# Second expert's rows gathered by quarters and turned by VectorE in a fused attention, gated layer and top-2 expert kernel

## The chip, the cores and the metric

One core of one Trainium2 chip runs the whole program in one launch. The metric is device time in microseconds (us), the median of several executions. The engines are TensorE (PE, with its weight loads as PEld), VectorE (DVE), ScalarE (ACT), GpSimd (POOL) and SyncE (SP), which here only issues transfers. Each runs its own instruction list in order; they meet at semaphores.

## What is computed

```python
x = attention(q, k, v)                      # window 64, 2304 rows of 512
x = (sigmoid(x @ w_gate) * (x @ w_val)) @ w_out
logits = x @ moe2_w_gate + log1p(exp(x @ moe2_w_noise)) * noise
top2 = the two largest of 8 logits, weights by softmax of the two
for e in range(8):                          # w1[e]: 512x1024, w2[e]: 1024x512
    out[rows of e] += weight * (relu(x[rows of e] @ w1[e]) @ w2[e])
```

## The kernel before, in words

Every float32 product is made of three TensorE products. Each operand is split into a high part, rounded by ScalarE, and a low part, the rest, subtracted by VectorE, and high by high, high by low and low by high are added up in PSUM.

The first stage (some 520 us) does the attention and the gated layer in 9 groups of 256 rows and 12 chunks each (GROUPS, FC; LAST is 108 chunks). The router decides for each group which rows go to which expert; GpSimd writes each row's number and weight into the table `places` in DRAM (`place_rows`).

The second stage goes over 8 experts (e). An expert has room for 5 tiles of 128 rows (TILES): tiles 0 to 2 are half p = 0 (368 columns are used), tiles 3 and 4 half p = 1 (256). What doesn't fit goes into left-over tiles after all experts. For each expert TensorE runs `up(e, p, f)` for 8 chunks f of 128 hidden columns (12 matmuls each), and `down(e, a)` for 5 tiles a (24 matmuls each). After each `up`, ScalarE's `relu` (line 1384) makes the high part of the hidden chunk, VectorE's `hidden_low` (L1732) the low part; `up(f)` needs the `hidden_low` of chunk f - 2, since two PSUM banks alternate. After each `down`, ScalarE's `rows_out` (L1394) scales the tile by the row weights, and GpSimd's `scatter` (L793) adds it to `out`.

An expert's weights come in 8 units of 128x1024 (n = 0 to 3 is w1, 4 to 7 is w2) through 4 raw buffers. SyncE loads them (`load_expert`), ScalarE's `high` (L1362) and VectorE's `low` (L1711) split them. There are two copies of the split w1 and one of w2: units 4 to 7 of expert 1 may be written only after the last `down` of expert 0, and the first `down` of expert 1 waits for all 8 (`e_lo`).

The rows of a tile are gathered by GpSimd with an indirect transfer (`gather(n)`) into one of two buffers `x_g`, and have to be turned, columns to partitions. There are two ways:

- Tiles of experts 0 and 1 (n < SQUARES = 10): one gather of whole rows (L779), then `turn_g(n)` on TensorE, four 128x128 transposes into PSUM (L1086). `xt_high` (L1374) and `xt_low` (L1725) split them from there.
- Tiles of experts 2 to 7: four gathers of quarter rows (L774), one for each quarter of the tile's rows, by a table `tab_q` whose row numbers VectorE has turned into quarter numbers (L1836 to L1838). VectorE's `turn_rows(n)` (L1719) transposes 32x32 blocks into the SBUF tile `x_t` (`v_nat1`). The w1 of such an expert is loaded by four transfers a unit (L577), so that its rows stand in the matching order.

The first two experts are interleaved. The order of the tiles is `ORDER = [0, 1, 2, 5, 6, 7, 3, 4, 8, 9]`, then 10 and on, where tile number is 5e + a; n counts places in this order. TensorE's list from the end of the first stage is `up(0,0)`, then `turn_g(3)`, `down(0,0)`, `turn_g(4)`, `down(0,1)`, `turn_g(5)`, `down(0,2)`; `up(1,0)` with `turn_g(6)` after f = 4 and `turn_g(7)` after f = 6; `up(0,1)`; `turn_g(8)`, `down(0,3)`, `turn_g(9)`, `down(0,4)`; `up(1,1)`; five `down(1,a)`; and from expert 2 on `up(e,0)`, `up(e,1)` and five `down` in turn. The orders on the other engines are written out by hand in the same way. During `up(1,1)` units 4 to 7 of expert 1 are split after f = 0, 2, 4 and 6. Before it VectorE works out the count of left-over tiles, a chain of 17 small instructions (L1846 to L1864).

GpSimd's list around this place: `place_rows(7)`, `gather(3)`, `gather(4)`; after the loop `place_rows(8)` (the last group), `gather(5)`, `scatter(0)`, `gather(6)`, `scatter(1)`, `gather(7)`, `scatter(2)`, `gather(8)`, `gather(9)`, `gather(10)`, `scatter(3)`, and so on. `gather(n)` waits until tile n - 2 is turned; `gather(5)` waits for the store of the last group's rows, which SyncE issues (`store_y`, L563) once gathers 0 to 4 have landed.

Of the kernel before, what the change touches and what calls it, by code (L numbers as in the profile page):

```python
# [13 lines left out]
P = 128  # L14


def attention_two_moe_program(nc, q, k, v, gv, w_out, r_gate, r_noise, noise, w1, w2, out):
# [61 lines left out]
    SQUARES = AHEAD * TILES  # L79
# [8 lines left out]
    UNITS = 8  # L88
    UW = 2 * EXW // UNITS
# [6 lines left out]
    with ExitStack() as ctx:  # L96
# [36 lines left out]
        tab_q = shared[:, 0:8 * (NE - AHEAD) * TILES].bitcast(I32).rearrange("p (b e n w) -> p b e n w", b=4, n=TILES, w=2)  # L133
# [38 lines left out]
        quarter = sb("quarter", [P, 1], I32)  # L172
        idx_r = sb("idx_r", [P, 1], I32)
# [168 lines left out]
        tab_q_in = sem("tab_q_in")  # L342
        quarters_done = sem("quarters_done")
# [30 lines left out]
        def turned_at(n):  # L374

            return ps_xt.rearrange("p (k m) -> p k m", k=KC) if n < SQUARES else x_t

        def turn_no(m):
            return ORDER.index(m)

        def loads(q):

            return 16 * sum(4 if i // UNITS >= AHEAD and i % UNITS < KC else 1 for i in range(q % 4, q + 1, 4))

        def gathers(n):

            return 16 * sum(1 if i < SQUARES else 4 for i in range(n % 2, n + 1, 2))

# [119 lines left out]
        def _(sp):  # L508
# [99 lines left out]
            for s in range(LAST + 2):  # L608
# [46 lines left out]
            for u in range(2):  # L655
                sp.wait_ge(gathered[u], 16 * ((5 + 1 - u) // 2))
# [3 lines left out]
            by_quarter = places.rearrange("(b c e n) w -> c b e (n w)", b=4, c=Q4, e=NE)[:, :, AHEAD:NE, 0:2 * TILES]  # L660
# [15 lines left out]
        def _(pool):  # L676
# [78 lines left out]
            def gather(n):  # L755
# [12 lines left out]
                if n >= SQUARES:  # L768
                    if n == SQUARES:
                        pool.wait_ge(quarters_done, 1)  # L770
                    pool.nop(nofuse=True)
                    e, a = divmod(m, TILES)
                    for b in range(4):
                        pool.indirect_dma_start(x_g[:, n % 2, b * P:(b + 1) * P], None, x2_quarters,  # L774
                                                bass.IndirectOffsetOnAxis(tab_q[:, b, e - AHEAD, a, 0:1], 0)
                                                ).then_inc(gathered[n % 2], 16)
# [57 lines left out]

            place_rows(GROUPS - 1)
            gather(5)
# [42 lines left out]
        def _(pe):  # L879
# [318 lines left out]
            for a in range(HEAD):  # L1198
                turn_g(3 + a)
# [7 lines left out]
            turn_g(8)  # L1207
            down(0, 3)
            turn_g(9)
# [38 lines left out]
        def _(act):  # L1248
# [679 lines left out]
```

## Time and profile before

| | |
|---|---|
| median of 3 runs | 983.2 us (982.27 to 983.57) |
| the profiled execution | 981.25 us |
| its span, first to last instruction | 979.0 us |
| TensorE busy | 968.5 us, 99% of the span |
| VectorE, ScalarE, GpSimd busy | 512.5, 370.1, 400.1 us |
| granted TensorE clock, mean | 0.999 of full |

The profile is of one execution. Its own time, 981.25 us, is the span and 2.25 us around it; the runs that are compared by their median are other executions. The chain of waits is followed back from the last instruction: a piece of it that is not a matmul is time in which TensorE stood still for somebody. A timeline row is one instruction, or several of a kind in a row, with the idle time of the engine before it in brackets, and what ended it. Ends of matmuls are modelled: consecutive pieces overlap by some 0.16 us in the timeline, not in the chain.

### The profile page before, as it was taken

Reading aid. Unit: us, or ns where it says so; the run is one execution under the profiler, and the core shown is the slowest. Engines: PE = TensorE matmul, PEld = TensorE weight load, DVE = VectorE, ACT = ScalarE, POOL = GpSimd, SP = SyncE. Lnnn points to the kernel's source line nnn. Section 1 sums busy time; section 2 is a strip of 40 time slices with the busy share of each in tenths; the row PEclk is TensorE's granted clock in tenths of the full one; section 3 lists DMA queues with packets and bytes.
Section 4 is the critical chain, followed back from the end, with each engine's and each line's share of the span. In section 5 each row is a group of like instructions: output and inputs, shape, how many; then the busy total and the mean of one; then the engine's idle time right before and its main releaser. Section 6 shows DMA issues by size and latency. Waiting matters only on the chain.

```text
span 979.0 us, 17644 instructions
## 1 busy us (share of the span) xinstructions
PE 968.5 (99%) x6503; PEld 853.5 (87%) x6503; DVE 512.5 (52%) x1277; ACT 370.1 (38%) x892; POOL 400.1 (41%) x401
## 2 busy tenths in 40 slices
PE   8999999999999999999999999999999999999997
PEld 7998888888888888888999898798998989898995
DVE  5565576665757576664554535543534434443420
ACT  6553343433334343423244423343433334343411
POOL 4882224242332424331212414663828284664402
PEclk9999999999999999999999999999999999999999
DMA  6756333243534324232044443672636466482503
GB/s 223 230 177 167 118 112 107 89 141 94 149 99 133 103 72 135 77 97 86 23 119 130 56 128 75 167 166 74 154 85 139 109 150 129 114 165 76 96 2 52
DMA packets 82727, 113.09 MB, mean 116 GB/s; under 512 B 19216, under 2 KB 45840, under 8 KB 82640
## 3 DMA queue, kind: packets, MB, share of 16 engines
q1 hardware_dynamic: 69008, 84.63, 29.5%
q0 software_dynamic: 13344, 27.05, 13.9%
q8 instruction: 53, 0.87, 0.4%
q14 instruction: 34, 0.28, 0.1%
q10 hardware_dynamic: 288, 0.26, 0.1%
HBM read 83.13 MB, written 28.77 MB: 114 GB/s over the span
## 4 chain that ended last, share of the span: by engine, by line
PE 98%; issue 0%; ACT 0%; DVE 0%; POOL 0%; POOLq 0%; ACTq 0%
PE bank L1118 22%; PE bank L1102 22%; PE bank L995 16%; PE bank L1018 16%; PE bank L1001 10%; PE bank L999 5%; PE bank L975 2%; PE bank L913 2%; PE bank L1125 1%; PE bank L1086 0%; PE bank L1044 0%; PE bank L1053 0%; PE bank L931 0%; PE bank L1066 0%; DVE wr L1711 0%
## 5 line engine op out<-in xcount | busy, mean ns | idle before, releaser
L1001 PE MATMUL bank<-xr,wr 128*128 128x256 f32 x864 | 242.7, 281 | 0.0
L995 PE MATMUL bank<-xr,wr 128*128 128x512 f32 x672 | 240.2, 397 | 0.0
L1102 PE MATMUL bank<-wr 128*128 128x256 f32 (+1 forms) x1536 | 223.6, 306 | 0.6 <-DVE xr L1732 0.5
L1102 PEld LDWEIGHTS bank<-wr 128*128 128x128 f32 x1536 | 221.1, 190 | 2.1 <-DVE xr L1732 1.0
L774 POOL DMA_INDIRECT arena<-x_rows,shared x120 | 129.7, 1081 | 145.6 <-DVE v_nat L1719 97.4
L1018 PE MATMUL bank<-wr,hr 128*128 128x512 f32 x648 | 170.6, 398 | 0.0
L742 POOL TENSOR_TENSOR hr<-arena,hr 128x256 fp32r<-128x256 f32 x84 | 62.0, 738 | 263.7 <-ACT hr L1315 263.7
L1001 PEld LDWEIGHTS bank<-xr,wr 128*128 128x128 f32 x864 | 163.6, 189 | 3.4
L995 PEld LDWEIGHTS bank<-xr,wr 128*128 128x128 f32 x672 | 126.2, 188 | 30.3
L1018 PEld LDWEIGHTS bank<-wr,hr 128*128 128x128 f32 x648 | 114.0, 188 | 23.3 <-issue 0.2
L1118 PE MATMUL bank<-wr 128*128 128x512 f32 (+1 forms) x576 | 133.2, 391 | 0.9 <-DVE wr L1711 0.9
L1118 PEld LDWEIGHTS bank<-wr 128*128 128x128 f32 (+1 forms) x576 | 104.9, 183 | 25.8 <-DVE wr L1711 1.1
L1315 ACT CAST hr<-arena 128x256 fp32r<-128x256 f32 x108 | 43.9, 407 | 133.3 <-DVE arena L1603 129.5
L1588 DVE TENSOR_REDUCE arena<-bank 128x256 f32<-128x512 f32 x84 | 58.1, 692 | 63.2 <-PE bank L1001 57.8
L1118 PE MATMUL bank<-wr,xr 128*128 128x512 f32 x384 | 88.8, 390 | 0.0
L1711 DVE TENSOR_TENSOR wr<-arena,wr 128x1024 fp32r<-128x1024 f32 x64 | 77.2, 1210 | 15.4 <-ACT wr L1362 11.3
L1118 PEld LDWEIGHTS bank<-wr,xr 128*128 128x128 f32 x384 | 71.9, 188 | 15.0
L1593 DVE TENSOR_REDUCE arena<-bank 128x256 f32<-128x512 f32 x84 | 58.0, 691 | 47.8 <-PE bank L1001 44.8
L1308 ACT ACTIVATE arena<-arena 128x256 f32<-128x256 f32 x84 | 35.0, 416 | 125.8 <-DVE arena L1588 125.3
L793 POOL DMA_INDIRECT out<-arena,tab x34 | 56.4, 1659 | 58.2 <-ACT arena L1394 51.2
L1394 ACT ACTIVATE arena<-bank,tab 128x512 f32<-128x512 f32 (+1 forms) x34 | 23.5, 690 | 133.7 <-PE bank L1118 106.8
L999 PE MATMUL bank<-xr,wr 128*128 128x256 f32 x384 | 70.1, 283 | 0.4 <-issue 0.4
(158 smaller groups left out, 1022.2 us busy)
## 6 DMA issues: line engine op xcount, KB each, us to landing
arena<-moe_w SPq DMA_DIRECT2D x40, 512.0 KB
arena<-moe_w SPq DMA_DIRECT2D x96, 128.0 KB
p_rows<-arena SPq DMA_DIRECT2D x28, 256.0 KB, 2.0
v_nat<-p_rows SPq DMA_DIRECT2D x112, 64.0 KB
arena<-gv SPq DMA_DIRECT2D x12, 512.0 KB, 4.5
out<-zeros POOLq DMA_DIRECT2D x20, 256.0 KB, 2.8
x_rows<-arena SPq DMA_DIRECT2D x9, 512.0 KB, 3.8
arena<-k SPq DMA_DIRECT2D x17, 256.0 KB, 4.9
```

What stands on the lines that cost most here:

```text
L742: pool.tensor_tensor(hr[:, r, 1], gate[:, 0], hr[:, r, 0].bitcast(F32), ALU.subtract).then_inc(h_lo, 1)
L774: pool.indirect_dma_start(x_g[:, n % 2, b * P:(b + 1) * P], None, x2_quarters, bass.IndirectOffsetOnAxis(tab_q[:, b, e - AHEAD, a, 0:1], 0 ...
L793: pool.indirect_dma_start(out[:, :], bass.IndirectOffsetOnAxis(row_no(m)[0:n], 0), y_s[0:n, m % 2], None, compute_op=ALU.add).then_inc(sca ...
L995: pe.matmul(ps_g[m].rearrange("p (a n) -> p a n", a=2), gv_w[:, f, m, kk], xr[:, g % 2, :, kk], start=(kk == 0), stop=False, skip_group_ch ...
L999: pe.matmul(ps_g[m][:, 0:GT], gv_w[:, f, m, kk], xr[:, g % 2, x, kk], start=(kk + x == 0), stop=False, skip_group_check=True)
L1001: mm = pe.matmul(ps_g[m][:, 0:GT], gv_w[:, f, 2 + m, kk], xr[:, g % 2, 0, kk], start=False, stop=(kk == KC - 1), skip_group_check=True)
L1018: mm = pe.matmul(ps_y[t], hr[:, f % 2, a, t * P:(t + 1) * P], wo_w[:, b, f], start=(f == 0 and n == 0), stop=(f == FC - 1 and n == 2))
L1102: mm = pe.matmul(ps_h[u % 2][:, 0:n], w1_r[e % 2][:, a, kk, f * P:(f + 1) * P], xT[p][:, b, kk, 0:n], start=(kk + x == 0), stop=(kk == KC ...
L1118: mm = pe.matmul(ps_e[m % 2][0:n], hT[p][:, i, f, cols.start:cols.start + n], w2_r[:, j, f], start=(f + x == 0), stop=(f == F2C - 1 and x ...
L1588: dve.tensor_reduce(gate[:, 0], ps_g[0].rearrange("p (a n) -> p n a", a=2), AX.X, ALU.add).then_inc(gates_added, 1)
L1593: dve.tensor_reduce(gate[:, 1], ps_g[1].rearrange("p (a n) -> p n a", a=2), AX.X, ALU.add).then_inc(vals_added, 1)
L1711: dve.tensor_tensor(unit(e, n, 1), raw[:, n % 4], unit(e, n, 0).bitcast(F32), ALU.subtract).then_inc(e_lo, 1)
```

## The change

Expert 1's tiles too now go the way of experts 2 to 7: quarter gathers, `turn_rows` on VectorE, w1 loaded by quarters. `SQUARES` becomes the first expert of this kind, and `squared(n)` tells which places in the order are meant: n = 3, 4, 5, 8, 9. The row numbers of its first three tiles come early in a table of their own, by four more transfers, and VectorE turns them into quarter numbers in chunk LAST - 5. `gather(5)` moves ahead of `place_rows(8)`. The rest of the quarter numbers is made one loop of 8 `hidden_low` earlier, and `gather(8)` waits for it. The left-over count moves behind the whole of VectorE's expert work. The last units of expert 1's weights are split after f = 0, 1, 3 and 5, and in every expert from 1 on ScalarE runs `xt_high` of the next expert's tile ahead of `rows_out`. For e = 0 and tiles 3 and 4 (n = 6, 7) nothing changes.

```diff
-    SQUARES = AHEAD * TILES
+    SQUARES = 1
+    LAST_UNITS = [0, 1, 3, 5]
+        tab_q_first = sb("tab_q_first", [P, 4, HEAD, 2], I32)
         def turned_at(n):
-            return ps_xt.rearrange("p (k m) -> p k m", k=KC) if n < SQUARES else x_t
+            return x_t if squared(n) else ps_xt.rearrange("p (k m) -> p k m", k=KC)
+        def squared(n):
+            return ORDER[n] // TILES >= SQUARES
@@ load_expert @@
-                if n < KC and e >= AHEAD:
+                if n < KC and e >= SQUARES:
@@ SyncE @@
+                    for j in range(4):
+                        sp.dma_start(tab_q_first[j * Q4:(j + 1) * Q4].rearrange("p b n w -> p b (n w)"),
+                                     places.rearrange("(b c e n) w -> c b e (n w)", b=4, c=Q4, e=NE)[:, :, SQUARES, 0:2 * HEAD]
+                                     ).then_inc(tab_q_first_in, 16)
                     for n in range(4, UNITS):
                         load_expert(0, n)
...
             for u in range(2):
-                sp.wait_ge(gathered[u], 16 * ((5 + 1 - u) // 2))
+                sp.wait_ge(gathered[u], gathers(4 - u))
             store_y(GROUPS - 1)
...
-            by_quarter = places.rearrange("(b c e n) w -> c b e (n w)", b=4, c=Q4, e=NE)[:, :, AHEAD:NE, 0:2 * TILES]
+            by_quarter = places.rearrange("(b c e n) w -> c b e (n w)", b=4, c=Q4, e=NE)[:, :, SQUARES:NE, 0:2 * TILES]
@@ GpSimd, gather(n) @@
-                if n >= SQUARES:
-                    if n == SQUARES:
+                if squared(n):
+                    if n == HEAD:
+                        pool.wait_ge(quarters_first, 1)
+                    if n == AHEAD * HEAD + LATE:
                         pool.wait_ge(quarters_done, 1)
                     pool.nop(nofuse=True)
                     e, a = divmod(m, TILES)
                     for b in range(4):
+                        no = tab_q_first[:, b, a, 0:1] if is_early(m) else tab_q[:, b, e - SQUARES, a, 0:1]
...
+            gather(5)
             place_rows(GROUPS - 1)
-            gather(5)
             scatter(0)
@@ TensorE @@
             for a in range(HEAD):
-                turn_g(3 + a)
                 down(0, a)
...
             for f in range(F2C):
                 up(0, 1, f)
-            turn_g(8)
             down(0, 3)
-            turn_g(9)
             down(0, 4)
@@ ScalarE @@
-                if f % 2 == 0:
-                    high(1, KC + f // 2)
+                if f in LAST_UNITS:
+                    high(1, KC + LAST_UNITS.index(f))
             for a in range(TILES):
                 if a < KC:
                     high(AHEAD, a)
+                xt_high(AHEAD * TILES + a)
                 rows_out(1, a)
-                xt_high(SQUARES + a)
...
                     if e < NE - 1 and a < KC:
                         high(e + 1, a)
-                    rows_out(e, a)
                     if e < NE - 1:
                         xt_high(TILES * (e + 1) + a)
+                    rows_out(e, a)
@@ VectorE @@
             def turn_rows(n):
                 dve.wait_ge(gathered[n % 2], gathers(n))
-                if n > SQUARES:
-                    dve.wait_ge(xt_hi, n)
-                    dve.wait_ge(xt_lo, n)
+                dve.wait_ge(xt_hi, n)
+                dve.wait_ge(xt_lo, n)
...
+                if s == LAST - 5:
+                    dve.wait_ge(tab_q_first_in, 16 * 4)
+                    link(dve.tensor_scalar(quarter[:], quarter[:], 5, None, ALU.arith_shift_right))
+                    to_quarters(tab_q_first[:].rearrange("p b n w -> p (b n) w")[:, :, 0]).then_inc(quarters_first, 1)
...
             hidden_low(0, 0, 2)
+            turn_rows(HEAD)
             copy_logits(GROUPS - 1)
...
             for a in range(HEAD):
-                xt_low(3 + a)
+                xt_low(HEAD + a)
+                if a + 1 < HEAD:
+                    turn_rows(HEAD + a + 1)
                 low(1, a)
...
                 hidden_low(1, 0, f)
                 if f in (4, 6):
                     xt_low(f // 2 + 4)
+            dve.wait_ge(tab_q_in, 16 * 16)
+            to_quarters(tab_q[:].rearrange("p b e n w -> p (b e n) w")[:, :, 0]).then_inc(quarters_done, 1)
             for f in range(F2C):
                 hidden_low(0, 1, f)
+                if f == 4:
+                    turn_rows(8)
-            dve.wait_ge(tab_q_in, 16 * 16)
-            link(dve.tensor_scalar(quarter[:], quarter[:], 5, None, ALU.arith_shift_right))
...
             xt_low(8)
+            turn_rows(9)
             xt_low(9)
...
             for f in range(F2C):
                 hidden_low(1, 1, f)
-                if f % 2 == 0:
-                    low(1, KC + f // 2)
+                if f in LAST_UNITS:
+                    low(1, KC + LAST_UNITS.index(f))
```

## Rows read from the trace of the kernel before

**Rows 1.** The page: the chain that ended last, by engine
```profile
PE 98%; issue 0%; ACT 0%; DVE 0%; POOL 0%; POOLq 0%; ACTq 0%
```

**Rows 2.** The chain in order of time: start us, us, what
```profile
544.40 0.44 PE bank L1086 x4
...
562.17 10.00 PE bank L1102 x60
...
596.91 5.51 PE bank L1118 x24
...
643.43 27.51 PE bank L1102 x192
...
945.11 27.29 PE bank L1118 x120
```

**Rows 3.** Timeline of TensorE: start us, us, instruction, idle before
```profile
576.82 13.75 PE L1102 MATMUL bank<-wr 128*128 128x368 f32 x108
...
602.25 4.47 PE L1102 MATMUL bank<-wr 128*128 128x256 f32 x36
...
615.89 16.67 PE L1118 MATMUL bank<-wr 128*128 128x512 f32 x72 [0.88 <-DVE wr L1711]
```

**Rows 4.** Timeline of ScalarE in up(1,1)
```profile
603.88 0.38 ACT L1384 ACTIVATE xr<-bank 128x256 fp32r<-128x256 f32 x1 [0.74 <-issue]
604.16 1.04 ACT L1362 CAST wr<-arena 128x1024 fp32r<-128x1024 f32 x1
606.28 0.38 ACT L1384 ACTIVATE xr<-bank 128x256 fp32r<-128x256 f32 x1 [1.08 <-PE bank L1102]
```

**Rows 5.** Timeline of VectorE in up(1,1)
```profile
604.29 0.42 DVE L1732 SCALAR_TENSOR_TENSOR xr<-bank,xr 128x256 fp32r<-128x256 f32 x1 [0.51 <-ACT xr L1384]
605.23 1.23 DVE L1711 TENSOR_TENSOR wr<-arena,wr 128x1024 fp32r<-128x1024 f32 x1 [0.51 <-issue]
...
614.61 1.22 DVE L1711 TENSOR_TENSOR wr<-arena,wr 128x1024 fp32r<-128x1024 f32 x1 [0.51 <-ACT wr L1362]
```

**Rows 6.** Timeline of VectorE from expert 0's first downs to the left-over count
```profile
559.56 1.22 DVE L1711 TENSOR_TENSOR wr<-arena,wr 128x1024 fp32r<-128x1024 f32 x1
...
579.61 0.54 DVE L1732 SCALAR_TENSOR_TENSOR wr<-bank,wr 128x368 fp32r<-128x368 f32 x1 [1.19 <-ACT wr L1384]
...
586.70 0.42 DVE L1732 SCALAR_TENSOR_TENSOR xr<-bank,xr 128x256 fp32r<-128x256 f32 x1 [1.01 <-ACT xr L1384]
...
591.54 0.29 DVE L1838 SCALAR_TENSOR_TENSOR shared<-shared,quarter 128x120 int32<-128x120 int32 x1
...
598.32 0.16 DVE L1846 CAST arena<-steps_i 128x14 f32<-128x14 int32 x1
```

**Rows 7.** Timeline of GpSimd: gathers and the last group's places
```profile
518.42 0.99 POOL L779 DMA_INDIRECT arena<-x_rows,tab_first  x1 [0.30 <-issue]
...
546.61 1.01 POOL L752 DMA_INDIRECT places<-pairs,slot_i  x1 [25.31 <-DVE pairs L1697]
...
592.57 0.95 POOL L774 DMA_INDIRECT arena<-x_rows,shared  x1 [13.77 <-DVE shared L1838]
...
596.32 0.95 POOL L774 DMA_INDIRECT arena<-x_rows,shared  x1 [0.30 <-issue]
...
637.67 0.95 POOL L774 DMA_INDIRECT arena<-x_rows,shared  x1 [0.30 <-issue]
...
651.30 1.67 POOL L774 DMA_INDIRECT arena<-x_rows,shared  x1 [0.30 <-issue]
```

**Rows 8.** Timeline of VectorE: the turn of expert 2's last tile
```profile
641.19 0.71 DVE L1719 STREAM_TRANSPOSE v_nat<-arena 128x512 f32<-128x512 f32 x1 [1.24 <-DMA arena<-x_rows,shared]
```

**Rows 9.** Busy time by stretch: us, PE, PEld, DVE, ACT, POOL, clock, DMA share, GB/s
```profile
598.60:600.00 1.40, 1.40 (x8) 1.15 (x7) 1.23 (x6) 0.00 (x0) 1.10 (x2) 1.00 0.00 0
```

**Rows 10.** Timeline of SyncE, and the page's landing time of such a store
```profile
529.36 0.38 SPq L563 DMA_DIRECT2D x_rows<-arena  x1
...
x_rows<-arena SPq DMA_DIRECT2D x9, 512.0 KB, 3.8
```

More of the change, by code:

```diff
@@ L342, in attention_two_moe_program @@
         tab_q_in = sem("tab_q_in")
+        tab_q_first_in = sem("tab_q_first_in")
+        quarters_first = sem("quarters_first")
         quarters_done = sem("quarters_done")
@@ L1711, in low, with to_quarters @@
                 dve.tensor_tensor(unit(e, n, 1), raw[:, n % 4], unit(e, n, 0).bitcast(F32), ALU.subtract).then_inc(e_lo, 1)
+            def to_quarters(numbers):
+                return dve.scalar_tensor_tensor(out=numbers, in0=numbers, scalar=4.0,
+                                                in1=quarter[:].broadcast_to(list(numbers.shape)), op0=ALU.mult, op1=ALU.add)
             def turn_rows(n):
                 dve.wait_ge(gathered[n % 2], gathers(n))
-                if n > SQUARES:
-                    dve.wait_ge(xt_hi, n)
-                    dve.wait_ge(xt_lo, n)
+                dve.wait_ge(xt_hi, n)
+                dve.wait_ge(xt_lo, n)
                 dve.nop(nofuse=True)
@@ L1830, in _ @@
                     xt_low(f // 2 + 4)
+            dve.wait_ge(tab_q_in, 16 * 16)
+            to_quarters(tab_q[:].rearrange("p b e n w -> p (b e n) w")[:, :, 0]).then_inc(quarters_done, 1)
             for f in range(F2C):
                 hidden_low(0, 1, f)
-            dve.wait_ge(tab_q_in, 16 * 16)
-            link(dve.tensor_scalar(quarter[:], quarter[:], 5, None, ALU.arith_shift_right))
-            q_rows = tab_q[:].rearrange("p b e n w -> p (b e n) w")[:, :, 0]
-            dve.scalar_tensor_tensor(out=q_rows, in0=q_rows, scalar=4.0, in1=quarter[:].broadcast_to([P, 4 * (NE - AHEAD) * TILES]),
-                                     op0=ALU.mult, op1=ALU.add).then_inc(quarters_done, 1)
+                if f == 4:
+                    turn_rows(8)
             xt_low(8)
+            turn_rows(9)
             xt_low(9)
+            for f in range(F2C):
+                hidden_low(1, 1, f)
+                if f in LAST_UNITS:
+                    low(1, KC + LAST_UNITS.index(f))
+            for a in range(TILES):
+                turn_rows(AHEAD * TILES + a)
+                if a < KC:
+                    low(AHEAD, a)
+                xt_low(AHEAD * TILES + a)
+            for e in range(AHEAD, NE):
+                for p in range(2):
+                    for f in range(F2C):
+                        hidden_low(e, p, f)
+                        if p == 0 and f < KC:
+                            low(e, KC + f)
+                for a in range(TILES):
+                    if e < NE - 1:
+                        turn_rows(TILES * (e + 1) + a)
+                    if e < NE - 1 and a < KC:
+                        low(e + 1, a)
+                    if e < NE - 1:
+                        xt_low(TILES * (e + 1) + a)
             rem, before, upto, share = (left[:, i] for i in range(4))
```

29 lines of the change are left out of this document (4 added, 25 removed).

## The prediction

> **What bounds the kernel.** I read the page's chain first: 98% of it is TensorE [rows 1]. A stall removed elsewhere is worth nothing; only TensorE's own work and its stops count. Then the chain in order of time around the change. From expert 2 on there is nothing to win: a half plus half of `up` takes 27.51 us and five `down` 27.29 us [rows 2], the same every time, so a matmul of 512 columns goes at 0.227 us, one `down` of 24 at 5.46, an `up` chunk of p = 1 at 1.44 (three in 4.47, with the 0.16 by which a timeline piece overlaps the next [rows 3]) and of p = 0 at (27.51 - 8 x 1.44) / 8 = 2.0. Third, TensorE's timeline of the one place that is slower than this: `up(1,1)` begins at 602.25 and the `down` behind it at 615.89 [rows 3], 13.64 us for eight chunks that need 11.52. So 2.12 us are lost there, 0.88 of them waiting for the last `low`. The clock is granted in full (0.999), and the engine is busy before and after the change alike, so I leave it there.
>
> **The change, part by part.**
>
> *Five turns leave TensorE.* From 544.40 to 562.17 stand three turns and three `down` [rows 2]: 17.77 - 3 x 5.46 = 1.39 us. From 590.57, the end of the piece that begins at 576.82 [rows 3], to 602.42, the end of the second `down` [rows 2], stand two and two: 11.85 - 10.92 = 0.93. Together 2.3 us (by the row of one turn, 0.44, it would be 2.2). All of it is on the path. `up(1,0)`, `up(0,1)` come 1.4 us earlier, `up(1,1)` 2.3.
>
> *The last units of expert 1 at f = 0, 1, 3, 5.* I run the same row durations forward, counting from the first matmul of `up(1,1)`. `relu(f)` starts 0.19 behind the end of its chunk, at 1.63 for f = 0; `high` 0.28 later and takes 1.04 [rows 4]; `hidden_low` starts 0.41 after `relu` and takes 0.44, `low` 1.23 [rows 5]. `low` of unit 4 then ends at 4.21, `hidden_low(1)` behind it at 4.57, so chunk 3, due at 4.32, starts at 4.61. Unit 5 ends at 5.7 and costs nothing. Unit 6 ends at 8.8, `hidden_low(4)` at 9.18, so chunk 6, due at 8.95 by then, starts at 9.22. Unit 7 ends at 11.72, before the last chunk does at 12.10. The first `down` starts at 12.1 in place of 13.64: 1.5 us. Both ends: 2.1 if no stop is left, and 0.9 if `relu(1)` is late again as it is now (606.28, where 605.3 was due by the chunks [rows 4]; what held it the trace does not say), since that shifts the same run to 12.77. I take 1.5, by the durations of the rows.
>
> *Gathers 3, 4 and 5 in four parts.* Four issues take 3 x 1.25 + 0.95 = 4.7 us (592.57 and 596.32 are the first and fourth), 0.3 apart from the next; in the dearest row one takes 1.67 [rows 7]. Gather 3 starts at 518.42 as before; gathers 3 and 4 are out by 528.4, or by 534 at 1.97 a part. SyncE issues sixteen loads for w1 where there were four, and four small table loads; then the store that stood at 529.36 and lands in 3.8 us [rows 10] goes at 531 to 537. `gather(5)` behind it is out by 540 to 549. Behind `gather(5)` GpSimd now has `place_rows(8)`, due at 546.61 [rows 7]: at worst 2 us late. What waits for that is the table, then `gather(6)`, needed by `turn_g(6)` at 572.17 - 1.4 [rows 2], 24 us after: four writes of 1.3, a table transfer and a gather at 3.8 each at most leave some 10 us. Nothing.
>
> *VectorE's turns*, 0.71 each [rows 8]. `turn_rows(4)` and `(5)` stand in waits for ScalarE's `rows_out`. What they must not delay is `low(1,3)`: it ended at 560.78 [rows 6] with `up(1,0)` at 562.17; it hangs on `down(0,1)`, which ends 0.93 us earlier, so 559.85 against 560.8 with 0.9 us left. `turn_rows(3)` and `(9)` have several us each. Nothing.
>
> *`gather(8)` and `turn_rows(8)`* is the tight place, since VectorE waits for the transfer with `hidden_low(0,1,5)` behind it, and TensorE's last chunk behind that. `hidden_low(1,0,7)` starts at 579.61 - 1.4 = 578.2 [rows 6], the quarter numbers are done at 579.05, GpSimd follows 0.74 later as it does now (591.83 to 592.57 [rows 6, 7]), the fourth issue ends at 584.5. Landing: at most 1.3 us later by one row (issue ended at 597.27, no traffic from 598.60 [rows 7, 9]), 2.6 by another, with other transfers beside it (issue ended at 638.62, turn released at 641.19 [rows 7, 8]). So 585.8 to 587.1. `turn_rows(8)` is due at 586.70 + 0.42 - 1.4 + 0.2 = 585.9 [rows 6]; TensorE's chunk 7 starts at 590.57 - 1.44 - 1.4 = 587.7, so a landing by 586.5 costs nothing and one at 587.1 costs 0.6. I take nothing: at 580 to 590 no weights are loading (the next load waits for `low(1,4)`), as in the row with 1.3.
>
> *The left-over count*, some 6 us (598.32 to 604.29 [rows 5, 6]), ended just in time for the first `hidden_low` of `up(1,1)`. It now runs from about 945, when TensorE begins its last 27.29 us [rows 2]; GpSimd asks for it ahead of the last but one scatter, some 20 us on. Nothing either way. *ScalarE's `xt_high` ahead of `rows_out`*: the fifth turn ends at 641.90 [rows 8], the copy by 642.6 if it takes as long, `down(1,4)` at 643.43 [rows 2]. Nothing, and nothing to gain, since these stages have no stop.
>
> Sum: 2.3 + 1.5 = 3.8 to 3.9 us. The profiled execution took 981.25 us (span 979.0 and 2.25 around it) and would take 977.4; the median of the runs, 983.2, lies 1.95 above it, so I say 979.3. A difference under 0.2%, 2 us, could not be told from none.
>
> **Rivals.**
>
> *The stop in `up(1,1)` stays* (0.15). Two units follow each other at f = 0 and 1, where VectorE has 1.23 + 0.44 = 1.67 us of work a chunk against TensorE's 1.44. With `relu(1)` late again it is 979.9; if all 2.1 us stay, 983.2 - 2.3 = 980.9.
>
> *`gather(8)` lands late* (0.08). For it: an issue of 1.67 with 0.3 behind it exists [rows 7]. Four such end at 587.4, landing at 590.0, 3.5 us past 586.5: 982.8. Against it: that row lies beside a `low`, and there is none at 580 to 585. The Trainium skill (GPSIMD Engine Reference, Specifications) says that GpSimd shares its SBUF interface with VectorE instructions that have two SBUF inputs, which a `low` has and a `hidden_low` has not; by that rule the long issues would stay away here, and the trace agrees so far, with 1.67 us beside a `low` and 0.95 without one.
>
> *VectorE's turns come onto the path* (0.03). If TensorE waited for each, 5 x 0.71 = 3.6 us would take the place of 2.3: 983.2 + 1.2 - 1.5 = 982.9. Against it: each has at least 0.9 us to spare above. The Trainium skill (VectorE: DVE Perf Modes, Rules for kernel authors) advises TensorE for a 128x128 transpose where PSUM will do as its target; by that advice the change would be given up and the 2.3 us stay in, and the time would be 981.7. The row speaks both ways: 0.71 us is longer than 0.44, but on an engine that is half idle.
>
> *Slower: `rows_out` held by `xt_high` in every expert* (0.05). ScalarE now waits for the fifth gather of the next expert before it frees a PSUM bank and starts the next `relu`. From the landing, turn, copy and `rows_out` (0.71 each at most), `relu` 0.4 and `hidden_low` 0.54 must end by chunk 2 of the next `up`, 643.43 + 4.0; from 641.19 [rows 2, 8] that leaves 3.1 us. If the gather lands 4.6 us later than now, 1.5 us are lost in each of six experts: 983.2 - 3.9 + 9 = 988.3. It decides from 4.1 us on (six times 1.0). Against it: GpSimd's order there is unchanged and its work moves with TensorE.
>
> *The change does not do what it says* (0.03): if the turns stayed on TensorE, 983.2 less what the units bring, 981.7. The five calls are gone from its list.
>
> **Numbers.** The forecast has 0.66. Its own range is 978.7 (no stop left) to 980.2. The stop's rival reaches 980.9, half of the late gather 981.1; runs of one kernel spread by 0.7 us. 978.2 to 981.6 leaves out the full late gather, the VectorE rival and the slower one. Faster by over 0.2% (under 981.2): the forecast, the first rival nearly whole and part of the second, 0.81. Within: the rest of these, the third and the last, 0.14. Slower: 0.05.
>
> **What would show it.** No L1086 between 544 and 562 but `down` after `down` at 5.46, `up(1,0)` at 560.8; two `down` of 10.9 before `up(1,1)` at 599.9; 12.1 us from there to the next `down`, at 612.0, with pauses of 0.3 before chunks 3 and 6; `turn_rows(8)` at 586, at once followed by `hidden_low`; the stages from expert 2 on at 27.51 and 27.29. Wrong would be a stop of TensorE at 587.7, or `down(1,0)` after 613, or a stage of a later expert over 27.6.

## The result: slower in the recorded measurement, faster on half of the chips

| | before | after | ratio, 95% interval |
|---|---|---|---|
| recorded measurement, median us | 982.93 (982.24 to 983.57, 6 runs) | 991.12 (989.66 to 992.82, 6 runs) | 1.0091 [1.0078, 1.0103] |
| its profiled execution: us, span, clock | 981.25, 979.0, 0.999 | 992.82, 991.1, 0.992 | |
| chip 2 | 980.97 | 977.53 | 0.9968 [0.9956, 0.998] |
| chip 2, a second time | 980.79 | 976.81 | 0.9962 [0.9949, 0.9976] |
| chip 8 | 980.59 | 976.83 | 0.9959 [0.9939, 0.9978] |
| chip 3 | 986.07 | 997.12 | 1.0098 [1.0072, 1.0124] |

The prediction, 979.3 us, missed the recorded time by 12 us. The same kernel, unchanged, then ran on other chips, and there it stands either 3.4 to 4.0 us below the kernel before, as forecast, or 11 above it. So two questions have to be kept apart: what the edits bring, and what some chips take. (The numbers only tell the chips apart; that of the recorded measurement is not on record.)

**Where the time went in the recorded profile.** The chain in order of time of the changed kernel (start us, us, what):

```profile
525.85 5.91 issue
531.77 4.02 PE bank L1118 x12
535.79 2.25 PE bank L1034 x6
538.04 2.00 PE bank L1118 x12
...
554.93 16.39 PE bank L1134 x72
571.32 10.00 PE bank L1118 x60
...
598.52 3.28 issue
601.79 2.45 PE bank L1118 x12
604.25 11.68 PE bank L1134 x48
...
628.20 27.34 PE bank L1134 x120
```

What was forecast is there: three `down` without a turn between them take 16.39 (17.77 with the turns, [rows 2]), and the stages from 628.20 on are as before. But TensorE stops twice, for 5.91 us ahead of the first chunk of `up(0,0)` and for 3.28 ahead of the last chunk of `up(0,1)`, and behind each stop the same work is slow. Busy time by stretch, the columns as in [rows 9] (us, PE, PEld, DVE, ACT, POOL, clock, DMA share, GB/s):

```profile
526.00:531.70 5.70, 0.00 (x0) 0.00 (x0) 0.00 (x0) 0.38 (x1) 3.07 (x4) 0.91 0.84 209
531.70:538.00 6.30, 6.23 (x19) 5.79 (x20) 3.21 (x4) 2.30 (x3) 0.00 (x0) 0.54 0.28 87
598.60:601.70 3.10, 0.00 (x0) 0.00 (x0) 0.38 (x1) 0.38 (x1) 2.19 (x4) 1.00 0.14 42
601.70:606.00 4.30, 4.21 (x17) 3.80 (x18) 0.04 (x1) 0.00 (x0) 2.72 (x3) 0.60 0.20 60
```

The granted clock falls to the 1.2 GHz level once TensorE has stood still: 12 matmuls of 368 columns in 4.02 us where 2.00 is usual, the last chunk of `up(0,1)` in 2.45 where 1.44 is, and the two `down` in 11.68 where 10.91 is. The first stop costs 5.91 + 2.02 + 0.86 = 8.8 us, the second 3.28 + 1.01 + 0.77 = 5.1. Together 13.9 us; less the 3.8 forecast that is 10.1, where the medians differ by 8.2 and the two profiled executions by 11.6 (the profiled one of after also waits 1.8 us for a load at its start).

**What the stops wait for.** In both, ScalarE, VectorE and TensorE nearly stand still and move on together; of the engines only GpSimd works all the time, and issues gathers. In the first stop the sixteen loads of w1 run as well (DMA share 0.84), in the second hardly anything does (0.14), so those loads can't be what both have in common. GpSimd's timeline, the last of the 12 issues in a row of the first place (four `place_rows`, gathers 3 and 4), then of the 12 of the second place the first of gather 8 and the fourth of gathers 8, 9 and 10:

```profile
529.03 0.95 POOL L791 DMA_INDIRECT arena<-x_rows,tab_q_first  x1 [0.30 <-issue]
...
590.26 1.00 POOL L791 DMA_INDIRECT arena<-x_rows,shared  x1 [15.87 <-DVE shared L1729]
...
594.08 0.94 POOL L791 DMA_INDIRECT arena<-x_rows,shared  x1 [0.30 <-issue]
...
599.09 0.95 POOL L791 DMA_INDIRECT arena<-x_rows,shared  x1 [0.30 <-issue]
...
604.09 0.95 POOL L791 DMA_INDIRECT arena<-x_rows,shared  x1 [0.30 <-issue]
```

And ScalarE's timeline, the gate of the first place and the `relu` of the second:

```profile
531.24 0.38 ACT L1321 ACTIVATE arena<-bank 128x256 f32<-128x256 f32 x1 [7.42 <-issue]
...
595.92 0.39 ACT L1397 ACTIVATE xr<-bank 128x256 fp32r<-128x256 f32 x1 [1.55 <-PE bank L1118]
600.90 0.38 ACT L1397 ACTIVATE xr<-bank 128x256 fp32r<-128x256 f32 x1 [4.59 <-remote]
607.26 0.66 ACT L1397 ACTIVATE xr<-bank 128x256 fp32r<-128x256 f32 x2 [5.97 <-remote]
```

The `relu` at 607.26 handles two chunks at once. TensorE had ended the first of them at 598.52 (the chain above), 8.7 us earlier; the second ended at 604.25. The one at 600.90 belongs to the chunk before, done at 596.8. So TensorE's work was finished, and its semaphore increments reached the other engines late.

The trace settles that it is the increment and not ScalarE that is late, since it holds each change of a semaphore with its own time. The chunks that ended at 596.82, 598.52 and 604.25 changed theirs at 600.88, 607.24 and 607.36. Counted over whole programs, the traces of the recorded measurement (before and after) and of chips 1, 3 and 11 each hold 9 to 27 changes made by TensorE, of some 640, that come 0.1 us or more behind the end of the matmul; the traces of chips 2, 6 and 8 hold none, of 663. No change made by ScalarE or VectorE is that late in any trace, on either kind of chip. And each late one falls into a run of GpSimd's issues or within 3 us of its end. The kernel before has them too in the recorded measurement, up to 1.9 us late around its `place_rows` and gather 3.

At the second place the increments arrive about when a gather is through: the fourth issues of the three gathers end at 595.0, 600.0 and 605.0, the `relu` follow at 595.9, 600.9 and 607.3. At the first place it is the same with the gate of the last chunk of the feed-forward layer: TensorE is done with it by 524.5, ScalarE starts at 531.24, and the run of issues ends at 529.98; the first chunk of `up(0,0)` starts 0.5 us after the gate. At the second place `up(f)` needs `hidden_low(f - 2)`, which needs the increment. A chunk takes 1.44 us, and `relu` and `hidden_low` are through some 0.9 behind its end, so TensorE stands still as soon as an increment is more than some 0.5 us late.

This calls a row of the kernel before in question. `relu(1)` at 606.28 [rows 4], for a chunk that ended at 605.3, is a late increment too, just behind the four issues of a gather.

### The profile page after: what moved, and what is told of

Its sections match the earlier page's. It is cut to its first block, busy times and chain, and to the rows that moved or that the text cites. A ratio compares the mean times of both kernels' runs of the same rounds, so it can differ in the third digit from the quotient of the medians.

```text
span 991.1 us, 17647 instructions
## 1 busy us (share of the span) xinstructions
PE 971.0 (98%) x6483; PEld 855.4 (86%) x6483; DVE 516.0 (52%) x1283; ACT 372.1 (38%) x892; POOL 423.7 (43%) x416
## 4 chain that ended last, share of the span: by engine, by line
PE 97%; issue 1%; DMA 1%; ACT 0%; POOL 0%; SPq 0%; DVE 0%; POOLq 0%
PE bank L1118 23%; PE bank L1134 22%; PE bank L1011 16%; PE bank L1034 16%; PE bank L1017 10%; PE bank L1015 5%; PE bank L991 2%; PE bank L929 2%; DMA arena<-q 1%; PE bank L947 0%; PE bank L1060 0%; PE bank L1069 0%; PE bank L1082 0%; PE bank L1141 0%; PE bank L1102 0%
## 5 line engine op out<-in xcount | busy, mean ns | idle before, releaser
L1118 PE MATMUL bank<-wr 128*128 128x256 f32 (+1 forms) x1536 | 226.5, 308 | 9.4 <-issue 9.2
L1118 PEld LDWEIGHTS bank<-wr 128*128 128x128 f32 x1536 | 223.5, 191 | 11.4 <-issue 10.3
L791 POOL DMA_INDIRECT arena<-x_rows,shared x128 | 139.7, 1091 | 140.3 <-DVE v_nat L1737 87.6
L809 POOL DMA_INDIRECT out<-arena,tab x34 | 62.5, 1837 | 64.0 <-ACT arena L1407 55.8
L1750 DVE SCALAR_TENSOR_TENSOR wr<-bank,wr 128x368 fp32r<-128x368 f32 x64 | 34.5, 539 | 64.7 <-ACT wr L1397 54.2
```

Source lines behind the costliest of these rows:

```text
L809: pool.indirect_dma_start(out[:, :], bass.IndirectOffsetOnAxis(row_no(m)[0:n], 0), y_s[0:n, m % 2], None, compute_op=ALU.add).then_inc(sca ...
L1118: mm = pe.matmul(ps_h[u % 2][:, 0:n], w1_r[e % 2][:, a, kk, f * P:(f + 1) * P], xT[p][:, b, kk, 0:n], start=(kk + x == 0), stop=(kk == KC ...
```

## The experiments

Times are given as the kernel's median against the median of the kernel before on the same chip, in us, with the ratio and its interval.

### Three versions without the long runs of issues (chip 6)

`e1_whole_all` takes gathers 3, 4, 5, 8 and 9 of the changed kernel as one transfer each, `e2_whole_first` 3, 4 and 5; `e4_paced`, called the paced kernel below, keeps all parts and holds them apart.

```diff
                     pool.nop(nofuse=True)
+                    if n in (3, 4, 5, 8, 9):
+                        pool.indirect_dma_start(x_g[:, n % 2], None, x2_rows[:, :], bass.IndirectOffsetOnAxis(row_no(m), 0)
+                                                ).then_inc(gathered[n % 2], 16)
+                        return
                     e, a = divmod(m, TILES)
```

```diff
                 if s == LAST - 2:
+                    pool.wait_ge(up_done, 2)
                     gather(4)
...
-            for n in (8, 9, 10):
-                gather(n)
+            gather(8)
+            pool.wait_ge(up_done, F2C * (half_no(0, 1) + 1))
+            gather(9)
             scatter(3)
+            gather(10)
```

> The changed kernel, with gathers 3, 4, 5, 8 and 9 as one transfer each in place of four (VectorE still turns them, w1 of expert 1 is still loaded by quarters). Left out: the rows of expert 1 then stand in another order than its w1, so its part of the output is not the reference's; the work of every other engine is the same. Theory A (a long run of GpSimd's indirect transfers, 12 without a pause, holds back the increments of TensorE's semaphores, and TensorE stops): both stops go, and the turns and the better order stay won: about 979. Rival B (the stops come from the sixteen w1 loads, or from the order of ScalarE and VectorE): the time stays near 991. Rival C (a dip of the granted clock that is there anyway, and the stop follows it): near 991.

> The same for gathers 3, 4 and 5 alone; 8 and 9 stay in four parts (the rows of three tiles of expert 1 then stand in another order than its w1: their part of the output is not the reference's). Theory A: the first stop (525.85 to 531.77 and the slow clock behind it, some 8 us) goes, the second (598.52 to 601.79, and the slow clock behind it, some 5 us) stays: 983 to 985. Rivals B and C: 991.

> The changed kernel with all its transfers, but broken up: gather 4 waits until TensorE has done two chunks of up(0,0), gather 9 until the last chunk of up(0,1), and gather 10 goes behind scatter 3. The number and form of the transfers is the changed kernel's. Theory A: the runs are 8, 4, 4 and 4 long and both stops nearly go: 979 to 982. Rival D (the quarter form itself costs, whatever the pauses): it stays within 2 us of 991. Rival B: 991.

Measured: 976.92 against 980.62, 0.9963 [0.9949, 0.9977]; 976.92, 0.9959 [0.9945, 0.9973]; 978.1, 0.9967 [0.9953, 0.9981]. None has a stop at the two places. Theory A fits e1 and e4 but not e2, which keeps 12 issues in a row at 581 to 596 and yet takes the same time. Such a result asks whether the changed kernel itself has the stops on this chip. It was not run on chip 6, and no trace of chip 6 has a late increment, so these three say nothing for or against theory A.

A fourth, `e3_before_spares`, the kernel before with 14 spare quarter gathers that nobody uses, gave no result: its extra tile needs 7168 bytes of a partition, and 2652 are free. `e6` below puts the same question to the kernel before in another way.

### The changed kernel again, and the quarter gathers alone (chip 2)

> The changed kernel as it is, beside the runs of before on one chip. The three variants run so far all lost the stops, even the one that kept gathers 8 and 9 in four parts, which theory A did not expect. Theory A (a long run of transfers holds back TensorE's increments): 989 to 992 with both stops, and the second one follows from the first in some way. Rival E (the stops are not the kernel's but those of one chip or one build, and were in that measurement alone): 976 to 978, as the variants.

977.53 against 980.97, 0.9968 [0.9956, 0.998]: rival E, the stops are not the kernel's alone. With nothing held back, the chain shows each step of the forecast. First the changed kernel, then the one before on the same chip (`e7_before_again`):

```profile
544.70 16.39 PE bank L1134 x72
561.09 9.99 PE bank L1118 x60
...
589.47 10.91 PE bank L1134 x48
600.38 1.45 PE bank L1118 x12
...
612.65 27.28 PE bank L1134 x120
639.93 27.51 PE bank L1118 x192
```

```profile
544.06 0.44 PE bank L1086 x4
...
561.83 10.00 PE bank L1102 x60
...
590.22 0.44 PE bank L1086 x4
...
602.07 1.45 PE bank L1102 x12
...
615.18 27.57 PE bank L1118 x120
```

> The kernel of before, for its profile on the same chip: whether TensorE's increments come late there during the four place_rows and gather 3 (0.8 to 1.9 us in the first profile of before) and in up(1,1). Theory A: as in the first profile. Rival E: no such lag on this chip.

The turns: 17.77 to 16.39 and 11.85 to 10.91, 1.38 + 0.94 = 2.3 us. `up(1,1)`: 13.11 to 12.27, 0.84 us. Sum 3.2. Some 0.5 us more lies outside the span: executions of the kernel before take 2.2 us beyond theirs, of the changed one 1.7 (981.07 and 978.8, 977.19 and 975.5); what makes that difference was not looked into. In this profile of before `up(1,1)` takes 13.11, not the 13.64 of [rows 3]: the missing 0.5 is the late increment of [rows 4], which isn't there here.

`e6_before_quarters` is the kernel of before with

```diff
+                if n in (3, 4, 5, 8, 9):
+                    for b in range(4):
+                        pool.indirect_dma_start(x_g[:, n % 2, b * P:(b + 1) * P], None, x2_quarters,
+                                                bass.IndirectOffsetOnAxis(row_no(m), 0)).then_inc(gathered[n % 2], 16)
+                    return
```

> The kernel of before with gathers 3, 4, 5, 8 and 9 as four transfers each, and nothing else changed: TensorE still turns them, w1 is loaded as before. Left out: the rows in x_g are then not those of the tile, so expert 1's part of the output is not the reference's; the work is the same. Theory A: the stops come up here too, about 8 to 12 us: 989 to 993. Rival E, or that the stops need the sixteen w1 loads as well: 981 to 983.

984.39, 1.0032 [1.002, 1.0044]: slower, but by no stop of the kind above: the trace has no late increment. TensorE waits for the data of gather 5, which in this kernel stands behind `place_rows(8)` (waits of TensorE: us in total, times, longest):

```profile
PE bank L1091 <- DMA arena<-x_rows,tab_first: 2.6, 1, 2.6
```

The `down` behind that wait takes 7.14 us where 5.50 is usual (`e7`), at a granted clock of 0.53 and then 0.50. So a gather 5 in four parts comes too late at its old place, at least where TensorE still turns the tile ahead of `down(0,2)`. That points to the move of `gather(5)` ahead of `place_rows(8)`, which the prediction only priced as harmless, as a part that the four-part form needs. It is not shown for the changed kernel, where the move alone was never undone and where the tile is needed later, for `up(1,0)`.

### Single edits undone (chip 2) and done alone (chip 8)

`e8_changed_third` has no edit (its result is in the first table) and `e9_paced_again` is the paced kernel. `e10_units_back` and `e11_count_back` start from the changed kernel; `e11` moves the 17 instructions of the left-over count back, between the two lines shown. `e13_before_units` starts from the kernel before.

```diff
-    LAST_UNITS = [0, 1, 3, 5]
+    LAST_UNITS = [0, 2, 4, 6]
```

```diff
             xt_low(9)
+            rem, before, upto, share = (left[:, i] for i in range(4))
...
+            dve.tensor_copy(more_i[:], left_f).then_inc(left_done, 1)
             for f in range(F2C):
                 hidden_low(1, 1, f)
```

```diff
-                if f % 2 == 0:
-                    low(1, KC + f // 2)
+                if f in LAST_UNITS:
+                    low(1, KC + LAST_UNITS.index(f))
```

(The last with `LAST_UNITS = [0, 1, 3, 5]`, and `high` in the same way.)

> The changed kernel as it is, a third time, beside the three below on one chip. Theory E (the two stops belong to the conditions of the first measurement, in which TensorE's increments came late, and not to the kernel alone): 0.996 to 0.998 of before here as in the second measurement, unless the same conditions return; then 1.009 and the stops with it, and the next kernel tells whether pacing helps.

> The changed kernel with gather 4 held until two chunks of up(0,0), gather 9 until the last chunk of up(0,1), gather 10 behind scatter 3. Where the changed kernel has no stops: the same as it, within 1 us. Where it has them: theory A wants at least half of them gone.

> The changed kernel with the last four weight units of expert 1 back at f = 0, 2, 4, 6. By the prediction's step (1.5 us from the order of the units in up(1,1), 13.64 to 12.1): up(1,1) takes 13.6 again and the time is 1.5 us above the changed kernel's. Rival: the stop came from the left-over count that ended just ahead of the first hidden_low of up(1,1); then the units alone cost nothing, and the next kernel does.

> The changed kernel with the left-over count back ahead of up(1,1) on VectorE. It takes some 6 us from the end of xt_low(9), 596.9 in the second profile of the changed kernel, to about 602.9, and the first hidden_low of up(1,1) is due at 602.26 there: at most 0.7 us late, and the chunk behind it has 2.2 us to wait for anyway. The prediction's step (nothing either way): within 0.5 us of the changed kernel. Rival: the whole order shifts by it, and up(1,1) takes 1 to 2 us more.

> The kernel of before with one edit of the change, the last weight units of expert 1 at f = 0, 1, 3, 5. By the prediction's sum the units are worth 1.5 us and the turns 2.3: 0.9985 of before, 979.5. In the changed kernel they were worth 0.8 to 1.0; and in before the left-over count ends 0.5 us after the first relu of up(1,1) and VectorE gets unit 5 a chunk after that, so it may be down to 0.5 us: 980.4. A loss would say that the two edits need each other.

`e9_paced_again`: 976.86 against 980.79, 0.9961 [0.9946, 0.9977], beside 976.81 of the changed kernel: where increments are on time, pacing costs nothing and brings nothing. `e10`: 977.82, 1.0 us above the changed kernel, and its chain has `up(1,1)` at 13.11 again:

```profile
600.34 1.45 PE bank L1118 x12
...
613.45 27.55 PE bank L1134 x120
```

`e11`: 976.71, no difference. `e13`: 979.59 against 980.5, 0.9988 [0.9979, 0.9997]; `up(1,1)` takes 12.28 there too (one piece of 12.44 from 603.08, less the usual overlap of 0.16). The units are worth 0.84 us by themselves, the count's place nothing.

### Longer runs of issues (chip 8), small transfers and the order of rows_out (chip 1)

All three start from the changed kernel. `e12_longer_runs` calls `spare_parts` behind gather 4 and behind gather 9; `e16_small_transfers` adds 28 loads at each of the two places on SyncE's queue; `e17_order_back` turns ScalarE's order back from expert 1 on.

```diff
+                for i in range(8):
+                    pool.indirect_dma_start(spare[:, i], None, x2_rows.rearrange("n (a c) -> (n a) c", c=8),
+                                            bass.IndirectOffsetOnAxis(tab_first[:, 0, i % 3, 0:1], 0)).then_inc(spared, 16)
```

```diff
+            for i in range(28):
+                sp.dma_start(small[:, i], places.rearrange("(p n) w -> p n w", p=P)[:, 0]).then_inc(small_done, 16)
```

```diff
-                xt_high(AHEAD * TILES + a)
                 rows_out(1, a)
+                xt_high(AHEAD * TILES + a)
```

> The changed kernel with 16 small spare gathers (8 columns of 128 rows each, into a tile that nobody reads): 8 behind gather 4, so that GpSimd issues 20 transfers without a pause where there were 12, and 8 between gather 9 and gather 10, again 20 in a row. If the length of the run can hold back TensorE's increments on any chip (theory A in a weaker form: the chips of the later runs only stand more), stops come up behind 530 and behind 592, several us each: 981 or more. Theory E (length alone does nothing; it takes the conditions of the first measurement): within 1 us of the changed kernel, 0.996 to 0.998 of before.

> The changed kernel with 56 small transfers on SyncE's queue (one table column of 8 bytes a row into a tile that nobody reads): 28 behind the loads of w1 of expert 1, while GpSimd issues gathers 3 and 4, and 28 from the third chunk of up(0,1) on, while it issues gathers 8 to 10. Each ends in increments of a semaphore, so the traffic of increments is several times the changed kernel's. Theory F (what holds TensorE's increments back is the number of increments and records made at the same time): stops or late increments at one of the two places, over 980. Theory E (the conditions of the first measurement are not to be had by what the kernel does): no stop, up to 2 us above the changed kernel for loads and a store that come later on SyncE's queue.

> The changed kernel with ScalarE's rows_out ahead of xt_high again, from expert 1 on. By the prediction's step (nothing, as no stage from expert 2 on has a stop): within 0.5 us of the changed kernel, 0.996 of before. Rival: the new order is what keeps the stages at 27.5 and 27.3, and the old one costs time in each of six experts.

`e12`: 976.53 against 980.5, 0.9958 [0.9943, 0.9973]. Twenty issues in a row and more (24 at the first place) do nothing on this chip, so length alone is not the cause. `e14_changed_fourth` and `e15_paced_third`, the changed and the paced kernel without an edit, were meant to meet the first conditions again and fell on the same chip: 976.83 and 976.57 against 980.59, 0.9959 [0.9939, 0.9978] and 0.996 [0.994, 0.9979].

> The changed kernel as it is, a fourth time, to meet the conditions of the first measurement again. Met: 1.008 to 1.010 of before, a granted clock of 0.992 and two stops of TensorE at 525.9 and 598.5. Not met: 0.996 of before, no stop.

> The changed kernel with gathers 4, 9 and 10 held apart, beside it. If the conditions are met, theory A (the run of transfers holds TensorE's increments back) wants at least half of the 13 us of the stops gone, below 1.003 of before; if it stays at 1.009, the run's length has nothing to do with it. If they are not met: 0.996.

On chip 1 the conditions came back. `e16`: 995.09 (two runs) against 986.45, 1.0089 [1.0062, 1.0115]. `e17`: 996.33 (992.44 to 1000.26), 1.0113 [1.0069, 1.0158]. TensorE's waits in `e17`:

```profile
PE bank L1118 <- issue: 8.2, 3, 4.1
PE bank L1034 <- DVE hr L1623: 2.9, 1, 2.9
```

The kernel before takes 986.45 here, some 6 us more than on chips 2, 6 and 8. The stops stand at the two known places. `e16` has them with 56 more transfers and is no worse than `e17` without, so increments from SyncE's transfers don't add to it: theory F is not borne out.

The trace of `e16` also shows that a shorter run can be enough. At its second place gather 10 comes late, so gathers 8 and 9 stand by themselves, eight issues in a row from 589.15 to 598.90. TensorE's wait of 3.67 us falls wholly into them, from the end of a chunk at 595.72 on: the `relu` at 598.49 belongs to the chunk that ended at 594.28.

```profile
598.49 0.38 ACT L1405 ACTIVATE xr<-bank 128x256 fp32r<-128x256 f32 x1 [5.22 <-issue]
...
599.39 2.53 PE L1126 MATMUL bank<-wr 128*128 128x256 f32 x12 [3.67 <-issue]
```

What `e17` was meant for can be read from its trace in spite of the stops: from `up(2,0)` to `up(3,0)` it is 54.80 us, 654.74 to 709.54, as in the changed kernel without stops (639.77 to 694.56 in `e5`). Five of the six later pairs of `up` take 27.68 us in the timeline, as there; one takes 28.26, and there three increments of TensorE are 0.4 to 1.2 us late. So the order of `rows_out` and `xt_high` costs nothing that can be seen beside that; its time on a chip without late increments was not measured.

```profile
654.74 27.68 PE L1118 MATMUL bank<-wr 128*128 128x368 f32 x192
...
709.54 27.68 PE L1118 MATMUL bank<-wr 128*128 128x368 f32 x192
...
764.33 28.26 PE L1118 MATMUL bank<-wr 128*128 128x368 f32 x192
```

### The paced and the changed kernel where increments are late (chips 11 and 3)

> The changed kernel with gathers 4, 9 and 10 held apart, once more, on whatever chip comes. The conditions of the first measurement belong to a chip, as the last call showed (stops at the same two places, 1.009 and 1.011 of before). On such a chip theory A (the run of 12 transfers sets the stops) wants this kernel without most of them: below 1.003 of before. If it stays above 1.007, GpSimd's transfers hold TensorE's increments back however they are spaced. On a chip as the others: 0.996.

> The changed kernel as it is, for the comparison with the paced one on a chip where TensorE's increments are seen to come late (the last call met one: they lag by 0.8 to 1.8 us in the paced kernel too, and it still stood at 0.9973 of before). Theory A: on such a chip the changed kernel stands at 1.007 to 1.011, with stops of several us at 526 and at 598; paced, it has lost them. If it stands at 0.997 there, pacing is not what made the difference. On a chip as 2, 6 and 8: 0.996.

`e18`, the paced kernel, on chip 11: 979.8 against 982.2, 0.9973 [0.9961, 0.9984]. That this is a chip with late increments its own trace shows, at 604 to 614 (ScalarE):

```profile
605.76 0.38 ACT L1400 ACTIVATE xr<-bank 128x256 fp32r<-128x256 f32 x1
607.99 0.38 ACT L1400 ACTIVATE xr<-bank 128x256 fp32r<-128x256 f32 x1 [1.85 <-PE bank L1121]
610.20 0.38 ACT L1400 ACTIVATE xr<-bank 128x256 fp32r<-128x256 f32 x1 [0.90 <-PE bank L1121]
612.41 0.38 ACT L1400 ACTIVATE xr<-bank 128x256 fp32r<-128x256 f32 x1 [1.82 <-remote]
```

The last of these is 1.8 us behind the end of its chunk (610.6). Here gathers 10 and 11 now follow each other, eight issues from 599.38 to 610.20 with no scatter between them. But apart from 1.5 us for GpSimd near the end (`zeros`), which every trace has, no wait for another engine is longer than 1.1 us, and `up(1,1)` takes 13.66 us (601.38 to 615.04 in the chain), 1.4 more than on chip 2:

```profile
PE bank L1121 <- ACT arena L1324: 1.1, 1, 1.1
...
PE bank L1121 <- issue: 0.5, 1, 0.5
PE bank L1121 <- DVE xr L1753: 0.5, 1, 0.5
```

`e19`, the changed kernel, on chip 3: 997.12 against 986.07, 1.0098 [1.0072, 1.0124], with two stops of 6.8 and 6.9 us:

```profile
PE bank L1118 <- DVE xr L1750: 7.1, 2, 6.9
PE bank L1118 <- ACT arena L1321: 6.8, 1, 6.8
```

So where increments come late, the changed kernel has the stops both times (the recorded measurement and `e19`), and so have its variants `e16` and `e17`, while the paced one, with the same number of transfers in the same form, among them the sixteen loads of w1, was without them the one time that it met such a chip. That it is the length of the runs which decides is not shown. The two kernels didn't meet on one such chip: the kernel before stands at 982.2 on chip 11 and 982.9 in the recorded measurement, where the changed kernel took 991.1, which is the nearest pair, but at 986 on chips 1 and 3. And two things speak against a plain count. On chip 1 eight issues were enough for a stop of 3.67 us (`e16`), where eight on chip 11 brought waits of 0.5. And from expert 2 on GpSimd issues up to 25 transfers with pauses of only 0.3 us (630.45 to 669.58 in the recorded profile), yet no stop of this kind is found there, and the latest increment on record is 2.2 us late (`e17`). Those runs have a scatter after every four gathers, the runs at the two places have none; whether that makes the difference wasn't tried.

What makes the increments late on some chips stays open. One thing goes with it in every trace: the changes of semaphores in it, counted, number 14,177, 14,166 and 14,170 for the changed kernel on chips 2 and 8, but 11,730 in the recorded measurement and 11,584 on chip 3; 14,163 and 11,810 for the paced kernel on chips 2 and 11; 13,669 and 11,359 for the kernel before on chip 2 and in the recorded measurement. Where increments come late, a sixth of the records is missing, nearly all of them of landed transfers (2330 of 2447 in the recorded profile of the changed kernel, against `e5`). Every execution whose time stands here has its clock and span on record too, so it may be the recording that is slow on those chips and holds the engines up. The Trainium skill (NOTIFIC — the notification-queue block, 7.1 Overflow: three behaviours, one of which stalls the engine) states that the path that takes such records can stall the engine that produces them. No run here can show whether that is what happened, nor what the kernels take on those chips unrecorded; that wasn't tried.

## Why the prediction was wrong, and where it was right

*The step that failed is "Gathers 3, 4 and 5 in four parts … Nothing", and with it the same verdict for `gather(8)`.* Both priced the issues by GpSimd's own time and by when the data land, and both were right in that: gather 8's four issues run from 580.02 to 584.77 on chip 2 (forecast to 584.5), `turn_rows(8)` starts at 586.63 (forecast 585.9 to 587.1), and the last chunk is not late. What it took at nothing without a reason is what the issues do to other engines: while GpSimd issues them, TensorE's increments can come late. On the chip of the recorded measurement that cost 13.9 us, 5.9 + 3.3 in the two stops and 4.7 at the lower clock behind them, against the 3.8 that the edits bring. Why they come late on one chip and not on another, and what about the run of issues decides how late, stays open. No rival had this mechanism; the slower one (ScalarE's order, 988.3) was of the right sign and the wrong place: the recorded profile has its stages from expert 2 on at 27.5 and 27.3.

*A row had shown it.* The prediction wrote of `relu(1)` at 606.28 that "what held it the trace does not say", and took 0.5 us of it as given. A consumer that starts 1 us behind the end of its producer, while GpSimd issues, was the same effect at a small size.

*The turns, 2.3 us*: 1.38 + 0.94 on chip 2. Right, and so was the way there.

*The units, 1.5 us*: 0.84 where increments are on time (e5, e10 and e13 agree). The end was right (12.27 for 12.1) but the start was not: 0.5 of the 13.64 us belonged to the late increment. The two recorded profiles alone, 13.64 and 12.27, would give 1.37.

*The left-over count, nothing*: right (e11). *ScalarE's order, nothing*: nothing speaks against it (e17). *`gather(5)` ahead of `place_rows(8)`, nothing*: as a delay of `place_rows(8)` it cost nothing; that the four-part gather may need this move, as `e6` with its 3.4 us suggests, the prediction didn't see.

*The sum*: 3.8 to 3.9 forecast; 3.4 to 4.0 measured on chips 2 and 8, of which the traces account for 3.2 within the span and 0.5 outside it, which no term of the sum had. That the total agrees so well is in part luck: the units brought 0.7 less than forecast, and the 0.5 makes up for most of it. *The range*, 978.2 to 981.6, left no room for late increments. "Wrong would be a stop of TensorE at 587.7" named the second place; the stop there came from the signals and not from the landing.

## What to carry to other kernels

Before GpSimd's indirect transfers are split into more parts, look in the trace for consumers that start a microsecond or more behind the end of their producer while GpSimd issues; if there are any, try to keep the runs of issues short by a wait on work that must be done anyway, as in the paced kernel. It lost 1 to 1.4 us at a place on chip 11, where the changed kernel lost 5 to 9 in the recorded measurement, but eight in a row also cost 3.7 us on chip 1, so this is a thing to try and not a rule. It costs nothing elsewhere: it is level with the changed one on chips 2 and 8 (0.9961 and 0.996 of before) and stood at 0.9973 on the one chip with late increments that it met. When a change of 0.4% comes out at +0.9% with stops that no data dependence explains, run the same kernel on another chip before explaining it. A gather in four parts may need a place further ahead in GpSimd's list, as `e6` had it for gather 5; look for what waits for its landing.

## What the runs showed of the hardware

- TensorE's semaphore increments are on time in every trace of three chips (2, 6, 8) and late on others: up to 8.7 us in the recorded measurement, 9.1 on chips 1 and 3 (`e16`, `e19`), 3.4 on chip 11. They are late only while GpSimd issues indirect transfers back to back or within 3 us behind, and ScalarE's and VectorE's own increments are not late in the same traces. On the first kind of chip 20 issues in a row (e12) make no difference.
- The granted clock fell to the 1.2 GHz level behind a stop of 5.9 us and behind one of 3.3, and in `e6` behind a wait of 2.6; before each TensorE had been busy without a pause. Of 13.9 us lost, 4.7 were the clock.
- The kernel before differs by 6 us between chips (980.5 to 981.0 on 2, 6 and 8; 982.2 on 11; 986 on 1 and 3). A ratio holds for a kind of chip, not for all.
